# Attention and two expert stages in one kernel: ScalarE issues the spread of the softmax reciprocals

## The reference, cut to what matters

```python
batch, n_heads, seq, head_dim = (4, 8, 576, 64)
scores = scale * np.matmul(q, k.transpose(0, 1, 3, 2))
mask = block_i >= block_j                  # blocks of 64 rows
scores = np.where(mask, scores, -1000000000.0)
scores = scores - np.max(scores, axis=-1, keepdims=True)
attn = np.exp(scores)
attn = attn / (np.sum(attn, axis=-1, keepdims=True) + 1e-09)
x = np.matmul(attn, v)                     # then (2304, 512)
...
for e in range(E):                         # 4 experts, 512 -> 1024 -> 512
    h = np.maximum(x @ w1[e], 0.0)
    out += p[:, e:e + 1] * (h @ w2[e])
...                                        # then a last stage with softmax, layer norm
```

## Time and profile before

| | us |
|---|---|
| median of 3 runs | 1149.01 (1148.9 to 1150.24) |
| the profiled execution | 1149.17 |
| its span, first to last instruction | 1147.4 |
| TensorE busy | 1134.8 |
| VectorE busy | 632.1 |
| ScalarE busy | 429.7 |
| GpSimd busy | 418.4 |

### The profile page before, as it was taken

The page is one execution under the profiler, slowest core; times in us unless marked ns, Lnnn a source line. Parts: engine busy times, 40 slices in busy tenths (PEclk is TensorE's granted clock), DMA queues, the critical chain, the costliest instruction groups (busy, mean ns, idle before and its releaser), DMA issues.

```text
span 1147.4 us, 16738 instructions
## 1 busy us (share of the span) xinstructions
PE 1134.8 (99%) x6115; PEld 1019.1 (89%) x6115; DVE 632.1 (55%) x1139; ACT 429.7 (37%) x943; POOL 418.4 (36%) x402
## 2 busy tenths in 40 slices
PE   8999999999999999999999999999999999999998
PEld 7999998888899998899999889999988987888887
DVE  8999996443343534244533334443424478667765
ACT  7998985312233211123211113321112354433432
POOL 8999996618144000034300004400003463533330
PEclk9999999999999999999999999999999999999999
DMA  4766768974825031253304071504125100000001
GB/s 153 230 214 218 238 195 259 363 290 168 319 65 217 13 133 60 83 202 119 130 19 175 1 265 56 212 1 150 44 89 196 44 12 10 29 19 28 19 28 37
DMA packets 68342, 146.29 MB, mean 128 GB/s; under 512 B 6064, under 2 KB 34736, under 8 KB 68272
## 3 DMA queue, kind: packets, MB, share of 16 engines
q1 hardware_dynamic: 67840, 145.29, 36.2%
q10 hardware_dynamic: 432, 0.07, 0.0%
HBM read 114.60 MB, written 30.74 MB: 127 GB/s over the span
## 4 chain that ended last, share of the span: by engine, by line
PE 89%; DMA 4%; POOL 2%; DVE 2%; ACT 1%; issue 1%; SPq 0%; DVEq 0%; ACTq 0%; POOLq 0%
PE s L1749 36%; PE outp L1612 19%; PE s L1612 15%; PE ring L1612 11%; PE ring L1623 3%; DMA x_stash<-x_tmp 2%; PE outp L1656 2%; PE outp L1655 2%; PE ring L1880 1%; DMA xr<-x_stash 1%; POOL x_tmp L781 1%; PE s L1823 1%; DMA q_raw<-in_q 1%; DVE neg_max L1232 1%; DMA x_rows<-x_n 0%
## 5 line engine op out<-in xcount | busy, mean ns | idle before, releaser
L1749 PE MATMUL s<-xr,w1s 128*128 128x384 f32 x2016 | 359.4, 336 | 3.9 <-DMA xr<-x_stash 1.8
L1749 PEld LDWEIGHTS s<-xr,w1s 128*128 128x128 f32 x2016 | 350.6, 188 | 8.7 <-DMA xr<-x_stash 2.1
L1082 ACT ACTIVATE hid_h<-u 128x384 fp32r<-128x384 f32 x96 | 50.5, 526 | 370.3 <-DVE u L1435 344.5
L716 POOL TENSOR_TENSOR work<-work 128x256 f32<-128x256 f32 x20 | 14.8, 738 | 392.0 <-DMA work<-in_moe_w 267.1
L1390 DVE SCALAR_TENSOR_TENSOR hid_l<-s,hid_h 128x384 fp32r<-128x384 f32 x48 | 26.8, 558 | 125.1 <-ACT hid_h L1078 125.1
L1348 DVE TENSOR_TENSOR u<-s,m_b 128x384 f32<-128x384 f32 x24 | 13.4, 558 | 132.0 <-PE s L1749 132.0
L1749 PE MATMUL s<-w1s,yop_h 128*128 128x512 f32 x252 | 85.2, 399 | 0.3 <-issue 0.3
L1078 ACT ACTIVATE hid_h<-s 128x384 fp32r<-128x384 f32 x48 | 23.6, 491 | 155.3 <-PE s L1612 155.3
L918 ACT ACTIVATE pr<-s,neg_max 128x576 f32<-128x576 f32 (+2 forms) x144 | 76.2, 541 | 4.4 <-DVE neg_max L1232 2.2
L1612 PE MATMUL s<-k_h,qb 128*128 128x288 f32 (+8 forms) x320 | 76.1, 325 | 1.8 <-DVE k_l L1244 1.1
L1612 PE MATMUL outp<-w_h,hid_h 128*128 128x512 f32 x192 | 75.5, 393 | 0.0
(11 more groups left out here) (169 smaller groups left out, 2444.0 us busy)
## 6 DMA issues: line engine op xcount, KB each, us to landing
xr<-x_stash SPq DMA_DIRECT2D x77, 768.0 KB, 6.1
r_sb<-r_scratch SPq DMA_DIRECT2D x16, 576.0 KB, 4.3
x_rows<-x_n SPq DMA_DIRECT2D x32, 288.0 KB, 4.5
work<-x_rows SPq DMA_DIRECT2D x24, 384.0 KB, 5.7
x_stash<-x_tmp SPq DMA_DIRECT2D x12, 768.0 KB, 3.7
work<-in_moe_w SPq DMA_DIRECT2D x32, 256.0 KB, 3.9
stage<-in_moe_w SPq DMA_DIRECT2D x32, 256.0 KB, 5.3
x_stash<-xr SPq DMA_DIRECT2D x7, 768.0 KB, 9.5
```

What stands on the lines that cost most here:

```text
L716: pool.tensor_tensor(s1, a21, a22, ALU.add).then_inc(w1_sums, 1)
L1082: act.activation(hid[slot][0][:, :], source, ACT.Relu).then_inc(hid_high, 1)
L1749: last = pe.matmul(target, x, y, start=start and i == 0, stop=stop and i == 2, skip_group_check=True)
```

## The change

`spread_r` moves from SyncE's program to ScalarE's. In `step(p)` it stands behind `exp_scores(7, n)`, in `last_step(p)` behind `high(T67B)`. Its three waits go with it. The DMA is the same and is now in ScalarE's DMA queue, in which only `store_r` was before. SyncE's loop goes from load_q straight on.

```diff
@@ SyncE
-            def spread_r(p):
-                sp.wait_ge(r_written, 16 * (p + 1))
-                if p >= 1:
-                    sp.wait_ge(left_scaled, p)
-                    sp.wait_ge(right_scaled, 2 * p)
-                sp.dma_start(r_sb[:, :], r_dram.rearrange("h x -> (h x)").partition_broadcast(P)).then_inc(r_loaded, 16)
-
@@ SyncE, loop over the pairs
                 if p + 3 < PAIRS:
                     load_q(p + 3)
-                spread_r(p)
                 if p == 11:
                     load_x(0, 1, (1,))
@@ ScalarE
+            def spread_r(p):
+                act.wait_ge(r_written, 16 * (p + 1))
+                if p >= 1:
+                    act.wait_ge(left_scaled, p)
+                    act.wait_ge(right_scaled, 2 * p)
+                act.dma_start(r_sb[:, :], r_dram.rearrange("h x -> (h x)").partition_broadcast(P)).then_inc(r_loaded, 16)
+
@@ ScalarE, step
                 high(T67B, p, par)
                 exp_scores(7, n)
+                spread_r(p)
                 high(T45, p, par)
```

## The result

The changed kernel takes 1152.34 us (median of 16 runs, 1151.23 to 1155.38) against 1149.20 for the kernel before on the same chip (16 runs, 1147.36 to 1151.38): a ratio of 1.0028 with an interval of 1.0021 to 1.0035, or 3.1 us slower. I had said 1153.5. One profile of either kernel is a draw, and where this text gives a price for the whole kernel it uses the timed ratio. Two executions of the experiments, at a far lower clock (1601 us of the kernel before, 4902 us of e11), are left out of the ratios.

The account below looks back on a forecast made before the run. TensorE, busy 1134.8 of 1147.4 us, was taken as the bound, with event order inside a pair deciding. Terms 3.1 + 1.3 + 0.6 - 0.5 = 4.5 us gave 1153.7, or 1153.5 against the median; range 1149.5 to 1160.5.

Parts of the forecast that it names:

- Issue, price: On ScalarE before high(T45): issuing the spread delays it 0.39 us, bounds 0.1 and 0.6; 3.1 us summed over pairs.
- Rival 1: Hidden issue: costs ScalarE only 0.1 to 0.2 us, pair 9's write lands in time; +0.5 us, 1149.5; chance 0.20.
- Who waits for high(T45): VectorE's low(T45), then TensorE's T0123 turn: 0.39 us lost in each of five pairs, less in others; 3.1 us summed.
- r_written: In pair 9 ScalarE waits for the reciprocals' write, delaying high(T45) 1.97 us; 1.3 us taken, bounds 0 and 1.7.
- Late arrival: The spread starts later but VectorE has 5.5 us of room against at most 4.8 taken now; no cost.
- rival 2: The spread arrives late beside a store, taking 6 us: +7 us over 14 pairs on top of 4.5, 1160.5; chance 0.13.
- The sentence on the stores: SyncE's stores start about 0.4 us earlier, loads behind feed nobody who waits; worth about nothing except in two places.
- Last pair: Pair 15: load_x(1, 0) goes ahead of the spread, delaying TensorE's m5; 0.6 us taken, bounds 0 and 2.5.
- Given back: VectorE's 0.90 us wait in pair 9 goes, returning about 0.5 us of TensorE; later stages shift with the attention's end.
- Sum: Whole kernel: 3.1 + 1.3 + 0.6 - 0.5 = 4.5 us slower, 1153.7, or 1153.5 against the median.
- Rival 3: ScalarE's issues stand behind SyncE's of store_x, 0.5 us more in 15 pairs: +7.5 on 4.5, 1161; chance 0.06.
- Rival 4: Faster: freed queue brings the last pair's loads forward; at most 2.3 us gained, 1146.7; chance 0.06.

Follow-up runs that it names:

- e11: The kernel before with TensorE's turn of T0123 in pair 14 done five times, no DMA moved: 1150.51 us, ratio 1.0013.
- e7: The kernel before with two useless 4 KB DMAs issued from ScalarE at the spread's place in each of 15 pairs: 1149.40 us, ratio 0.9997.
- e6: The kernel before with ScalarE also waiting for the reciprocals' write in pair 9, issuing nothing: 1149.98 us, ratio 1.0003.
- e10: The changed kernel with pair 9's spread moved behind exp_scores(5) on ScalarE: 1152.73 us, ratio 1.0032 against the kernel before.
- e4: The kernel before with only pair 15's spread issued from ScalarE: 1150.68 us, ratio 1.0013.
- e5: The changed kernel with SyncE waiting for the write in pairs 9 and 15 before the store and load_x(1, 0): 1150.50 us, ratio 1.0007 against the kernel before.
- e2: The kernel before with only the spreads of pairs 9 and 15 issued from ScalarE: 1152.42 us, ratio 1.0030.
- e8: The changed kernel again, unedited, in a later session: 1153.62 us, ratio 1.0027 against the kernel before.
- e9: The changed kernel with the spreads of pairs 9, 12 and 15 kept on SyncE: 1149.68 us, ratio 1.0003 against the kernel before.
- e1: The changed kernel with the spreads of pairs 9 and 15 kept on SyncE: 1149.91 us, ratio 1.0013 against the kernel before.
- e3: The kernel before with only pair 9's spread issued from ScalarE: 1150.31 us, ratio 1.0013.

## Why the prediction was right, and where it was not

The time was 1.2 us from the forecast (3.1 us slower, where 4.5 was said), on the side and in the range given, but by terms that don't match. That the size came out is in large part luck: the largest term was paid nowhere, and terms put at nothing or too small filled its place.

- **Issue, price: wrong.** 3.1 us were charged, 0 were paid. The failed step is "It can start about 0.03 us after the start of the accumulator read". The lower bound named the reason ("if the sequencer works while the read runs"), and even that was too cautious: the sequencer goes through the waits and the issue as much as 1.3 us before the engine gets there (71.46 against 72.80). The gap of 0.13 us behind the write, taken as a price, was none: e7's thirty issues gave 0.9997. The trace of before had shown as much, as the write's issue runs beside an activation of the same length, and the gap stands behind both:

```profile
101.50 0.28 ACT L929 ACTIVATE pt_h<-ring 128x128 fp32r<-128x128 f32 x1
```

  Rival 1, with 0.1 to 0.2 us, was nearer, and then assumed that pair 9's write lands in time.
- **Who waits for high(T45): unused.** The chain through low(T45) to the turn is real: in pair 9 1.9 us of wait on ScalarE become 1.6 on TensorE. But in ordinary pairs nothing entered it.
- **r_written: the block right, its weight not.** 1.3 us forecast, 1.6 seen in the profile. Timed, the block alone (e6) is not to be told from nothing, and lifting it (e10) saves nothing; e10's profile has 1.3 us saved in the pair, so its weight stays open between these.
- **Late arrival, "I take no cost": wrong in the pairs that count.** In ordinary pairs it held: slower landings (median 4.9 us) found their room. The 5.5 us that I gave as the limit was passed in pairs 9 and 15, at 7.3 and 7.6, which is rival 2's mechanism in two pairs instead of fourteen. (Pair 3 passed it too, at 6.4, and VectorE did not wait.) The sentence on the stores said that their early start "is worth about nothing", and looked only at who waits for them, not at what must now queue behind them.
- **Last pair: right in kind, too small.** 0.6 us forecast, 1.8 measured (4.2 - 2.4, and 2.1 - 0.3 in e4). The rows in hand gave 4.3 + 2.8 = 7.1 us to the landing; it was 7.6. With 5.6 us of room that is 1.5 us, and I took less than half of it without a row that said so.
- **Given back: wrong place.** The 0.90 us of VectorE's wait in pair 9 did not go but grew to 1.95, as the data became later with the pair. What came back, 2.1 us in this profile, came behind 220 us, where I had written that later stages "shift with it". A fall of the clock behind a long wait, which the sum has no term for, worked the other way (last section).
- **Sum.** At the attention's end: 0 + 1.6 + 1.3 - 0.5 (pairs 10 to 14) + 1.8 = 4.2 us, close to the 4.5 forecast, then 2.0 at the end of this execution and 3.1 in the median. 3.1 us charged wrongly stood in for 2.5 us of late arrival (1.3 in pair 9, 1.2 more in pair 15).
- **Rival 3, a lock between two issuers: not seen.** The issues on ScalarE took 0.345 to 0.387 us, SyncE's took 0.33; nothing near the 0.5 us of extra that it needed. Of the 16, 15 were made while an issue of SyncE's was under way, pair 9's (0.345 us) inside one of 1.06 us, and the one that met none took 0.357. The Trainium skill's lock wait ("Perfetto Trace Analysis", section "DMA Instruction — HWDGE (DVE, Sync)"), a section that names only DVE's and SyncE's sequencers as the sharers, can't have been over a few hundredths of a microsecond here.
- **Rival 4, faster: excluded** by the time and by pair 15, which got 1.9 us longer. SyncE's wait on the scaling stayed and grew, as the store now bears it alone:

```profile
SPq L502 <- DVE x_n L1256: 83.0, 15, 10.7
```

It was 57.9 us. The load queue is not freed of this wait by the change: it waits for the scaling with its next item.

## What to carry to other kernels

A DMA in one queue with the loads has a place in the order, and its wait keeps others back; moved to another queue it loses both, so list what is now issued ahead of it, pair by pair, and compare the landing behind that with the room. A change that costs nothing measurable in thirteen pairs can be decided by two or three in which bulk traffic passes; look at those first. And don't charge a compute engine for issuing a DMA before checking in the trace whether the issue starts while the engine still computes.

## What the runs showed of the hardware

- ScalarE's sequencer runs ahead of its datapath through waits and DMA issues: 1.1 us of issues in one go (e7) left the engine's work in place. A wait that isn't yet met does stop it, and then what stands behind it (1.90 us in pair 9).
- A 4.5 KB write on its own queue took 4.9 us to land behind attention rows on the other (112.12 to 116.99), against at most 2.1 in pair 8 of the kernel before. The spread of 576 KB, issued by ScalarE behind SyncE's traffic, took 5.5 to 7.3 us in pair 9 and 7.2 to 8.2 in pair 15 (e5 apart, where SyncE is held), against 3.7 to 4.8 in the kernel before. Separate queues did not shield one from the other.
- Behind a wait of TensorE of 2.1 to 2.8 us in pair 9 the granted clock fell to 0.50 in some executions (e2, e6 and e8), and not in others: in e5 it stayed at 1.00 behind 2.45 us. e9 has it in another stage, behind a wait of 1.90 us for xr, where TensorE goes from 2.0 to 4.0 us late, and its profiled execution is the longest of its runs (windows with columns as in the earlier trace rows):

```profile
244.00:246.00 2.00, 1.11 (x6) 1.12 (x7) 0.00 (x0) 0.00 (x0) 0.00 (x0) 1.00 1.00 418
246.00:248.00 2.00, 2.00 (x9) 2.00 (x8) 0.56 (x1) 0.00 (x0) 0.00 (x0) 0.51 1.02 427
```

A late DMA on this kernel's path can so cost up to about twice its wait: in e6, T0123 starts 2.1 us late, and at its end and behind it TensorE is 3.6 late.
- How often the clock falls can be read from the mean granted clock of each execution, on record to three places. The four profiled executions with such a fall have 0.998 or 0.999, the nine others 1.000. It was below 1.000 in 11 of 16 and 6 of 8 executions of the changed kernel, 5 of 7 of e2 and 4 of 7 of e10, but in 3 of 31, 2 of 30 and 3 of 22 of the kernel before, none of 12 of e1, 1 of 11 of e9, and none to 4 of 10 or 11 in each of e3 to e7 and e11. In e8's session the two executions of the changed kernel at 1.000 took 1150.65 and 1151.21 us, the six others 1152.97 to 1154.88; in the first session the medians are 1151.91 and 1152.71. So part of the 3.1 us is probably the clock that falls behind the long waits, and not the waits themselves; how large a part is open, as the two sessions differ.
